# Token MLP of a mixer kernel: 576 tokens as four tiles of 128 and one of 64 in place of six of 96

## The reference

```python
def _moe2_ref(x, w_tok1, w_tok2, w_ch1, w_ch2):
    xt = x.transpose(0, 2, 1)
    h = np.maximum(xt @ w_tok1, 0.0) @ w_tok2
    u = x + h.transpose(0, 2, 1)
    h2 = np.maximum(u @ w_ch1, 0.0) @ w_ch2
    return (u + h2).astype(np.float32)
```

## Time and profile before

| what | value |
|---|---|
| median of three runs | 1030.07 us (1028.97 to 1031.05) |
| the profiled execution | 1031.78 us |
| its span, from the first to the last instruction | 1029.9 us |
| granted TensorE clock, mean | 0.993 |
| TensorE busy | 1011.4 us (98%) |
| VectorE, ScalarE, GpSimd busy | 389.6, 290.9 and 188.0 us |
| the token MLP on TensorE | from 649.18 to 718.23 us |

### The profile page before, as it was taken

The page is one execution under the profiler, slowest core; times in us unless marked ns, Lnnn a source line. Parts: engine busy times, 40 slices in busy tenths (PEclk is TensorE's granted clock), DMA queues, the critical chain, the costliest instruction groups (busy, mean ns, idle before and its releaser), DMA issues.

```text
span 1029.9 us, 18136 instructions
## 1 busy us (share of the span) xinstructions
PE 1011.4 (98%) x7731; PEld 905.8 (88%) x7731; DVE 389.6 (38%) x690; ACT 290.9 (28%) x580; POOL 188.0 (18%) x159
## 2 busy tenths in 40 slices
PE   7999999999999999999999999999999999999998
PEld 5999899888989999999899999777899999999997
DVE  4697887882241321322313213555121212121211
ACT  4765565563331111111111112353111111111110
POOL 2552635567910000000000000044100000000000
PEclk8999999999999999999999999999999999999999
DMA  5322242433601010010010210675101010101000
GB/s 163 109 74 74 74 119 70 137 114 109 189 1 62 1 61 1 1 61 0 0 61 0 68 33 1 183 254 215 33 3 59 3 60 2 59 2 60 3 29 31
DMA packets 47649, 66.34 MB, mean 64 GB/s; under 512 B 22432, under 2 KB 23392, under 8 KB 47456
## 3 DMA queue, kind: packets, MB, share of 16 engines
q1 hardware_dynamic: 45856, 59.10, 18.4%
q10 hardware_dynamic: 1728, 6.29, 1.7%
HBM read 46.51 MB, written 18.87 MB: 63 GB/s over the span
## 4 chain that ended last, share of the span: by engine, by line
PE 91%; DVE 4%; POOL 3%; ACT 1%; issue 1%; DMA 0%; SPq 0%; DVEq 0%; ACTq 0%; POOLq 0%
PE mlp_hid L984 11%; PE mlp_hid L982 11%; PE mlp_y L997 11%; PE mlp_y L998 11%; PE mlp_hid L983 11%; PE mlp_y L996 11%; PE num L316 3%; PE kv L302 3%; PE proj L273 2%; PE proj L275 1%; PE proj L274 1%; PE mlp_turn_in L967 1%; PE four L322 1%; PE tok_y L1261 1%; PE pt L288 1%; PE four L325 1%
## 5 line engine op out<-in xcount | busy, mean ns | idle before, releaser
L1096 DVE SCALAR_TENSOR_TENSOR mlp_h_lo<-mlp_hid,mlp_h_hi 128x384 fp32r<-128x384 f32 x168 | 93.6, 557 | 466.5 <-ACT mlp_h_hi L1028 466.5
L982 PE MATMUL mlp_hid<-mlp_ut_hi,mlp_w_hi 128*128 128x384 f32 x672 | 229.7, 342 | 2.4 <-POOL mlp_w_lo L944 2.4
L984 PE MATMUL mlp_hid<-mlp_ut_hi,mlp_w_lo 128*128 128x384 f32 x672 | 227.1, 338 | 0.0
L983 PE MATMUL mlp_hid<-mlp_ut_lo,mlp_w_hi 128*128 128x384 f32 x672 | 226.0, 336 | 0.0
L1028 ACT ACTIVATE mlp_h_hi<-mlp_hid 128x384 fp32r<-128x384 f32 x168 | 82.6, 492 | 505.1 <-PE mlp_hid L984 505.1
L998 PE MATMUL mlp_y<-mlp_w_hi,mlp_h_lo 128*128 128x512 f32 x504 | 199.4, 396 | 0.0
L997 PE MATMUL mlp_y<-mlp_w_lo,mlp_h_hi 128*128 128x512 f32 x504 | 199.1, 395 | 0.0
L996 PE MATMUL mlp_y<-mlp_w_hi,mlp_h_hi 128*128 128x512 f32 x504 | 197.4, 392 | 0.3 <-DVE mlp_h_lo L1096 0.2
L944 POOL TENSOR_TENSOR mlp_w_lo<-mlp_w_raw,mlp_w_hi 128x1024 fp32r<-128x1024 f32 x26 | 61.7, 2394 | 409.8 <-DVE tok_x_lo L1316 396.5
L982 PEld LDWEIGHTS mlp_hid<-mlp_ut_hi,mlp_w_hi 128*128 128x128 f32 x672 | 126.6, 188 | 8.3 <-issue 2.6
L983 PEld LDWEIGHTS mlp_hid<-mlp_ut_lo,mlp_w_hi 128*128 128x128 f32 x672 | 126.6, 188 | 5.3
(11 more groups left out here) (123 smaller groups left out, 1162.4 us busy)
## 6 DMA issues: line engine op xcount, KB each, us to landing
mlp_u<-u_scratch SPq DMA_DIRECT2D x12, 768.0 KB, 4.6
mlp_w_raw<-in_w_mlp SPq DMA_DIRECT2D x14, 512.0 KB, 4.5
mlp_w_raw<-in_w_mlp ACTq DMA_DIRECT2D x12, 512.0 KB, 7.4
v<-in_v SPq DMA_DIRECT2D x16, 320.0 KB, 3.7
...
x_scratch<-mlp_u SPq DMA_DIRECT2D x5, 768.0 KB, 3.5
```

The lines of the kernel that those rows point to most:

```text
L982: nc.tensor.matmul(out, w_hi[:, j, col], hi, start=(c == 0), stop=False)
L983: nc.tensor.matmul(out, w_hi[:, j, col], lo, start=False, stop=False)
L984: last = nc.tensor.matmul(out, w_lo[:, nf - 1 - j, col], hi, start=False, stop=(c == DC - 1))
L1096: nc.vector.scalar_tensor_tensor(out=h_lo[:, j % 2, :], in0=hid[j % 2][:, 0:BT], scalar=0.0, in1=h_hi[:, j % 2, :], op0=ALU.max, op1=ALU.s ...
```

## The change

The token tiles become `FULL` = 4 tiles of 128 and one of `LEFT` = 64, `KT` = 5 in all, in every step of the token MLP: the loads of w1 and x, their casts and low halves, both layers, the adds and the stores. Tensors that held 96 x 6 rows hold 128 x 5; `rows_of(t)` cuts the last tile to 64 partitions. The first layer's weights of the last tile are 64 rows x 128 columns, the second layer's 128 rows x 64 columns. Each load of w1 and of x, and each store, becomes two transfers, one of the four full tiles and one of the 64 tokens; the store of the full tiles waits for their adds only. `w1` is cast and subtracted in two instructions instead of one. Counts on semaphores go by `KT`, `TURN` becomes 1, so that the first transposes stand behind tile 1, and GpSimd's waits become `KT * (b + 2)`.

```diff
+FULL, LEFT = S // 128, S % 128
+KT = FULL + 1
...
-    x_one = sb("x_one", [T, NT, D])
+    x_one = sb("x_one", [128, KT, D])
...
+    def rows_of(t):
+        return slice(0, 128 if t < FULL else LEFT)
...
-            sp.wait_ge(stored[0], 16)
-        sp.dma_start(x[b][:, :, :], src[b].rearrange("t p d -> p t d")).then_inc(x_loaded[b], 16)
+            sp.wait_ge(stored[0], 32)
+        tokens = src[b].rearrange("t p d -> (t p) d")
+        sp.dma_start(x[b][:, 0:FULL, :], in_tiles(tokens)).then_inc(x_loaded[b], 16)
+        sp.dma_start(x[b][0:LEFT, FULL, :], tokens[128 * FULL:S]).then_inc(x_loaded[b], 16)
...
-        sp.wait_ge(tile_done, NT * b + NT)
-        sp.dma_start(dst[b].rearrange("t p d -> p t d"), x[b][:, :, :]).then_inc(stored[b], 16)
+        tokens = dst[b].rearrange("t p d -> (t p) d")
+        sp.wait_ge(tile_done, KT * b + FULL)
+        sp.dma_start(in_tiles(tokens), x[b][:, 0:FULL, :]).then_inc(stored[b], 16)
+        sp.wait_ge(tile_done, KT * b + KT)
+        sp.dma_start(tokens[128 * FULL:S], x[b][0:LEFT, FULL, :]).then_inc(stored[b], 16)
...
-    FIRST = [(t, j) for t in range(NT - 2) for j in range(MT)] + [(t, j) for j in range(MT) for t in (NT - 2, NT - 1)]
+    FIRST = [(t, j) for t in range(KT - 2) for j in range(MT)] + [(t, j) for j in range(MT) for t in (KT - 2, KT - 1)]
-    SECOND = [(t, j) for j in range(MT) for t in range(3)] + [(t, j) for t in range(3, NT) for j in range(MT)]
+    SECOND = [(t, j) for j in range(MT) for t in range(3)] + [(t, j) for t in range(3, KT) for j in range(MT)]
...
-            last = passes(hid[j][:, :], w1_hi[:, t, cols], w1_lo[:, t, cols], x_hi[:, t, :], x_lo[:, t, :],
-                          t == 0, t == NT - 1)
+            k = rows_of(t)
+            last = passes(hid[j][:, :], w1_hi[k, t, cols], w1_lo[k, t, cols], x_hi[k, t, :], x_lo[k, t, :],
+                          t == 0, t == KT - 1)
...
-            cols = slice(T * t, T * t + T)
-            last = passes(y[t % 3][0:T, :], w2_hi[:, j, cols], w2_lo[:, j, cols], h_hi[:, j, :], h_lo[:, j, :],
+            cols = slice(128 * t, min(128 * t + 128, S))
+            last = passes(y[t % 3][rows_of(t), :], w2_hi[:, j, cols], w2_lo[:, j, cols], h_hi[:, j, :], h_lo[:, j, :],
...
-        nc.scalar.copy(w1_hi[:, :, :], w1[:, :, :]).then_inc(w_rounded, 1)
+        nc.scalar.copy(w1_hi[:, 0:FULL, :], w1[:, 0:FULL, :])
+        nc.scalar.copy(w1_hi[0:LEFT, FULL, :], w1[0:LEFT, FULL, :]).then_inc(w_rounded, 1)
...
-        TURN = NT - DC
+        TURN = KT - DC
...
-            mlp2["gpsimd"](pool, [(MLP2_CHUNKS[b][0], tok["x_split"], NT * (b + 2)) for b in range(B - 1)])
+            mlp2["gpsimd"](pool, [(MLP2_CHUNKS[b][0], tok["x_split"], KT * (b + 2)) for b in range(B - 1)])
```

More of the change, by code:

```diff
@@ L1194, in token_mlp @@
     w2_lo = sb("w2_lo", [128, MT, S], F32R)
-    x_one = sb("x_one", [T, NT, D])
+    x_one = sb("x_one", [128, KT, D])
     h_hi = sb("h_hi", [128, MT, D], F32R)
     h_lo = sb("h_lo", [128, MT, D], F32R)
-    x_hi = sb("x_hi", [T, NT, D], F32R)
-    x_lo = sb("x_lo", [T, NT, D], F32R)
+    x_hi = sb("x_hi", [128, KT, D], F32R)
+    x_lo = sb("x_lo", [128, KT, D], F32R)
     sb("second_mlp_weights", [128, HIGH - TOK_LOW])
     at = lambda n, shape, dt, offset: nc.alloc_sbuf_tensor_at(f"tok_{n}", shape, dt, offset=SBUF + 4 * HIGH + offset)
[L1203 to L1207, removed]
+    w1 = at("w1", [128, KT, TOK], F32, 0)
+    x_two = at("x_two", [128, KT, D], F32, 0)
+    w1_hi = at("w1_hi", [128, KT, TOK], F32R, 8 * TILES * D)
+    w1_lo = at("w1_lo", [128, KT, TOK], F32R, 8 * TILES * D + 4 * KT * TOK)
+    x_zero = at("x_zero", [128, KT, D], F32, 26464)
     x = (x_zero, x_one, x_two, x_zero)
@@ L1227, in token_mlp, with in_tiles @@
     stored = [sem(f"stored{b}") for b in range(B)]
+    def in_tiles(rows):
+        return rows[0:128 * FULL].rearrange("(t p) d -> p t d", p=128)
+    def rows_of(t):
+        return slice(0, 128 if t < FULL else LEFT)
     def sp_load(sp, b):
@@ L1254, in sync @@
         for b in range(3):
-            sp.wait_ge(stored[b], 16)
+            sp.wait_ge(stored[b], 32)
         before_last(sp)
         sp_store(sp, 3)
-        sp.wait_ge(stored[3], 16)
+        sp.wait_ge(stored[3], 32)
     def passes(out, lhs_hi, lhs_lo, rhs_hi, rhs_lo, start, stop):
@@ L1298, in pe_step, with act_split @@
                     aside(pe, t)
-    def act_split(act, b, tiles=range(NT)):
-        act.wait_ge(x_loaded[b], 16)
+    def act_split(act, b, tiles=range(KT)):
+        act.wait_ge(x_loaded[b], 32)
         wait_if(act, hid_done, MT * b)
         for t in tiles:
-            nc.scalar.copy(x_hi[:, t, :], x[b][:, t, :]).then_inc(x_rounded, 1)
+            nc.scalar.copy(x_hi[rows_of(t), t, :], x[b][rows_of(t), t, :]).then_inc(x_rounded, 1)
     def act_hidden(act, b):
-        wait_if(act, y_done, NT * b)
+        wait_if(act, y_done, KT * b)
         for j in range(MT):
@@ L1354, in vector_first @@
     def vector_first(dve, step):
-        if 1 <= step <= NT // 2:
-            dve_split(dve, 0, 2 * step - 2)
-            dve_split(dve, 0, 2 * step - 1)
+        if 1 <= step <= 3:
+            for t in range(KT)[2 * step - 2:2 * step]:
+                dve_split(dve, 0, t)
         if step:
@@ L1360, in vector_first @@
         dve.wait_ge(w_rounded, 1)
-        nc.vector.tensor_tensor(w1_lo[:, :, :], w1[:, :, :], w1_hi[:, :, :], ALU.subtract).then_inc(w_split, 1)
+        for k, t in ((slice(0, 128), slice(0, FULL)), (slice(0, LEFT), slice(FULL, KT))):
+            last = nc.vector.tensor_tensor(w1_lo[k, t, :], w1[k, t, :], w1_hi[k, t, :], ALU.subtract)
+        last.then_inc(w_split, 1)
     def vector(dve, aside):
@@ L1370, in vector @@
                 dve_split(dve, b + 1, 1)
-            for t in range(NT):
+            for t in range(KT):
                 dve_tile(dve, b, t)
```

27 lines of the change are left out of this document (15 added, 12 removed).

## The result

The changed kernel takes 1022.19 us in the median of four runs (1021.54 to 1024.02) against 1029.53 of the kernel before (1028.97 to 1031.05): a ratio of 0.9929, interval 0.9912 to 0.9947, so 7.3 us less (5.5 to 9.1). The forecast was 1022.5.

A forecast was written before the change was run, and what follows sets the result against it. TensorE was taken to bound the kernel, its matmuls setting the token MLP's time. Batch gains of 1.5 + 2.37 + 1.38 + 2.27 = 7.5 us off a median of 1030.07 gave 1022.5 us, range 1019.8 to 1025.5.

The forecast's parts named there:

- The price of a matmul: Token MLP on TensorE: 0.228 us each in the first layer, 0.234 in the second; fewer matmuls save 2.77 a batch.
- Switching: First layer's 64-row weights: entering and leaving them costs TensorE 0.35 us a batch (0 to 1.05), plus 0.05 for columns.
- Batch 1: Second batch of the token MLP: the full matmul saving less switching and columns, a gain of 2.37 us.
- Batch 2: Third batch: GpSimd's subtractions delay the add of tile 0, TensorE idles 1.25 us; gain 1.38 (0.6 to 2.6).
- Batch 3: Last batch: 2.37 us less a wait of 0.1 (0 to 1.2) for the next stage's load; gain 2.27.
- Batch 0: First batch: tied to VectorE through w2's low half; gain taken as 1.5 us (1.3 to 1.7).
- fewer matmuls in front leave w2 where it is: Batch 0: w2's low half keeps its time, 656.54, so the second layer starts only 0.29 us earlier.
- The tie itself: Batch 0: second layer starts 0.69 + 0.11 us behind the end of w2's low half, at 657.34.
- (a): Token MLP: batch 2 does not stall and switching is free; gain 10.2, 1019.8 us; chance 0.17, or towards it.
- (b): Token MLP: transfers and weight casts come late; gain only 4.1, 1025.9 us; chance 0.18.
- (c): Batch 2: the clock falls in TensorE's idle stretch, 1.3 us lost, 1023.8 us; chance 0.03.
- (d): 64-row and 64-column matmuls miss the full rate; at a quarter rate 1056 us; slower 0.04, about even 0.04.

The follow-up runs named there:

- e2: Changed kernel with 128-row weights for the last tile in the first layer, w1's rows 64 to 127 zero; 1020.98 us (0.9908).
- e10: The kernel of e3 unchanged, run again for a second trace; one run, 1020.14 us.
- e11: Changed kernel with each GpSimd subtraction of mlp2's weights cut into two half pieces; one run, 1020.86 us.
- e4: Changed kernel with two last-tile passes in one 128-row matmul, half 0 three tiles ahead, w2 split by halves, adds before splits; 1019.19 us (0.9881).
- e12: The kernel of e4 with VectorE adding two tiles, not one, before the first split of the next batch; 1021.89 us (0.9916).
- e1: Changed kernel with each batch's six 64-row-weight matmuls placed together, so two switches a batch instead of four; 1022.01 us (0.9906).
- e3: Changed kernel with VectorE's order altered: each split of the next batch's x follows the add of its own tile; 1020.85 us (0.9895).
- e9: The kernel of e1 unchanged, run again for a second trace; one run, 1019.68 us.
- e8: Changed kernel with w2 loaded behind the x of batch 1 on SyncE's queue; 1028.51 us.

## Why the prediction was right, and where it was not

**The price of a matmul** held: 0.228 us in the first layer and 0.23 in the second with 128 x 128 weights, and the 48 matmuls that went carry the gain.

**Switching**: the forecast took 0.35 us a batch with ends at 0 and 1.05. One switch by rows costs 0.20 (0.35 for an entry and exit was taken from the earlier trace rows, 0.40 was measured), columns cost nothing, and since the wait for the rounding now passes beside the switches, the net is 0.43 a batch by e2, where 0.40 was forecast with the columns. The rule that the Trainium skill, TensorEngine Tiling (Array Packing), Key Properties, gives, that a change of tiling mode drains TensorE, was weighed there: rows agree with it at 0.20 us a switch, the change to 64 columns shows no such cost.

**Batch 1**: 14.53 forecast, 14.47 measured.

**Batch 2**: 15.78 forecast, 15.78 measured, and for the reason given: GpSimd's end pins the add of tile 0, the fourth tile starts 12.89 into the batch (12.92 forecast), and one low half is blocked for 2.76 us (about 2 or more). The Trainium skill, SBUF — State Buffer, section SBUF: two separate sides, says that the first of the two holds the shared port for its whole instruction and the other blocks; the endings in e10 and e11, 0.55 us behind GpSimd's piece, agree. The order in e11 does not: the low half had begun 0.24 us ahead of GpSimd's half piece, and the half piece still went first. TensorE's idle time was forecast at 1.25 us; the profile shows 0.99, and by the distance of the starts (687.99 to 689.37, 0.23 usual) it is 1.15.

**Batch 3**: 15.86 forecast, 15.80 measured; the wait of 0.1 for the load did not come, since the store of the full tiles was issued before the batch began and the load started 4.27 in, not 5.2 to 6.6, and took 4.5 us, not 5.6. That the load is near the edge was right: e4 waits 0.41 for it, e12 2.92.

**Batch 0** is the term that was mis-sized: a gain of 1.5 (1.3 to 1.7) was forecast, 2.35 measured. The step that failed is "fewer matmuls in front leave w2 where it is": it took the arrival of one trace, 7.36 us from the batch's start to the end of w2's low half, for a constant. It was 6.82, 6.64 and 6.59 in the three traces of the changed kernel, and the second layer started 7.52 or 7.53 in, where the batches without w2 start it too. So batch 0 was bound by TensorE there (in the first trace the two tie), not by w2, and gained what the matmuls give, as batch 1 did. The tie itself was priced well: where w2 landed in 4.7 or 4.8 us the second layer did start 8.21 and 8.24 in, 8.16 forecast, 0.70 behind the low half (0.80 forecast). Why w2 came earlier than in the trace before is not shown.

So the stage gained 8.5 us, not 7.5. That the median fell 7.3 and met the forecast within 0.3 us is partly luck: the stretch ahead of the stage, which differs by up to 2.8 us between traces of one kernel, hid the difference. Against medians of the kernel before that were taken later (1030.51 of seven runs, 1030.22 of six) the changed kernel's 1022.19 is 8.0 to 8.3 less.

**The rivals**: (a) needed batch 2 free, and e10 shows what that gives, 1.3 us; (b) did not come in the changed kernel, but in e1 and e3 a late w2 and a late cast cost 0.6 and 1.1 us of the stage against the second traces, e9 and e10; (c) did not come at 0.99 us idle, and e8 shows it at 4.03; (d) falls with the 0.23 between 64-row matmuls (its 0.43 for a quarter of the rate would be 0.48 by the 0.12 of the earlier trace rows, which the 0.20 fits no better).
